# Layer 2's first step: five VectorE instructions and two ScalarE instructions change places

## The reference, cut to what matters

```python
x = attn_out.reshape(B * S, D)
h = x @ w_in;  g = h * np.cos(h);                          x = g @ w_out   # layer 1
h = x @ w_in2; g = h * np.clip(h + 3.0, 0.0, 6.0) / 6.0;   y = g @ w_out2  # layer 2
```

## Time and profile before

| | us |
|---|---|
| median of 3 runs | 1143.38 (1143.23 to 1143.67) |
| the profiled execution's own time | 1142.86 |
| its span, first to last instruction | 1140.9 |
| TensorE busy in the span | 1134.9 (99%) |
| ScalarE busy | 874.7 (77%) |
| VectorE busy | 808.4 (71%) |
| GpSimd busy | 786.5 (69%) |

### The profile page before, as it was taken

One profiled execution on the slowest core, in us unless ns is written; L12 is line 12 of the kernel. 1 busy time (PEld: TensorE's weight loads), 2 busy tenths in 40 slices (PEclk: granted clock), 3 DMA queues, 4 the chain that ended last, 5 costly groups with the idle time before them and its releaser, 6 DMA issues.

```text
span 1140.9 us, 16262 instructions
## 1 busy us (share of the span) xinstructions
PE 1134.9 (99%) x5350; PEld 960.9 (84%) x5350; DVE 808.4 (71%) x1120; ACT 874.7 (77%) x1457; POOL 786.5 (69%) x644
## 2 busy tenths in 40 slices
PE   9999999999999999999999999999999999999998
PEld 9888899888888888888888878888888888888898
DVE  6777856878888888888888887755555555555544
ACT  4777777778888888888889978767667677676665
POOL 0677677877868768768668999857557558557554
PEclk9999999999999999999999999999999999999999
DMA  9476465010020020020021210100100200200100
GB/s 348 120 226 188 144 208 195 15 48 9 1 74 1 1 74 1 1 74 1 18 76 56 91 59 1 38 37 1 61 14 1 75 1 1 70 1 1 38 1 32
DMA packets 44685, 68.47 MB, mean 60 GB/s; under 512 B 3497, under 2 KB 26761, under 8 KB 44602
## 3 DMA queue, kind: packets, MB, share of 16 engines
q1 hardware_dynamic: 44602, 67.43, 17.7%
HBM read 43.04 MB, written 24.48 MB: 59 GB/s over the span
## 4 chain that ended last, share of the span: by engine, by line
PE 97%; ACT 1%; DVE 1%; DMA 1%; issue 0%; SPq 0%; ACTq 0%; DVEq 0%
PE banks L762 41%; PE banks L740 36%; PE banks L698 3%; PE banks L718 3%; PE banks L669 2%; PE banks L612 2%; PE banks L617 2%; PE banks L613 2%; PE banks L575 2%; PE banks L636 1%; PE banks L633 1%; DMA xb<-in_x 1%; PE banks L639 0%; PE banks L651 0%; PE banks L652 0%; PE banks L654 0%
## 5 line engine op out<-in xcount | busy, mean ns | idle before, releaser
L1610 POOL TENSOR_TENSOR gb_lo<-gb,gbh 128x512 fp32r<-128x512 f32 (+1 forms) x352 | 465.4, 1333 | 264.1 <-ACT gbh L1120 261.5
L1120 ACT ACTIVATE gbh<-gb 128x512 fp32r<-128x512 f32 (+1 forms) x352 | 218.8, 621 | 74.1 <-DVE gb L1348 61.1
L762 PE MATMUL banks<-gbh,w1h 128*128 128x512 f32 (+1 forms) x704 | 272.5, 387 | 0.0
L762 PE MATMUL banks<-gb_lo,w1h 128*128 128x512 f32 (+1 forms) x704 | 272.5, 387 | 0.0
L762 PE MATMUL banks<-gbh,w_lo 128*128 128x512 f32 (+1 forms) x704 | 272.4, 387 | 0.0
L1348 DVE SCALAR_TENSOR_TENSOR gb<-gb,banks 128x512 f32<-128x512 f32 (+1 forms) x144 | 97.0, 673 | 134.9 <-ACT gb L1113 134.9
L762 PEld LDWEIGHTS banks<-gbh,w1h 128*128 128x128 f32 x704 | 132.1, 188 | 26.2 <-issue 0.3
L762 PEld LDWEIGHTS banks<-gb_lo,w1h 128*128 128x128 f32 x704 | 132.2, 188 | 25.9
L762 PEld LDWEIGHTS banks<-gbh,w_lo 128*128 128x128 f32 x704 | 132.1, 188 | 25.9
L1107 ACT ACTIVATE gb<-gb,half_pi 128x512 f32<-128x512 f32 x160 | 115.1, 720 | 33.8 <-DVE gb L1335 33.1
L740 PE MATMUL banks<-th,sh 128*128 128x512 f32 (+1 forms) x352 | 136.5, 388 | 0.0
(11 more groups left out here) (133 smaller groups left out, 2153.2 us busy)
## 6 DMA issues: line engine op xcount, KB each, us to landing
t<-x_spill SPq DMA_DIRECT2D x20, 512.0 KB, 4.7
w<-in_w_ff SPq DMA_DIRECT2D x32, 256.0 KB, 3.5
v<-y_spill SPq DMA_DIRECT2D x24, 260.0 KB
xb<-in_x SPq DMA_DIRECT2D x12, 512.0 KB, 9.8
dbs<-in_db SPq DMA_DIRECT2D x24, 256.0 KB, 2.7
y_spill<-y SPq DMA_DIRECT2D x24, 256.0 KB, 2.3
x_spill<-yt SPq DMA_DIRECT2D x10, 512.0 KB, 3.3
out_y<-yt SPq DMA_DIRECT2D x10, 512.0 KB, 3.1
```

What stands on the lines that cost most here:

```text
L762: mm = pe.matmul(bank[:, y_bank(tile) + c, 0:w], wt[:, at:at + P], a[:, 0:w], start=(p == 0 and e == 0 and n == 0), stop=(p == PAIRS - 1 a ...
L1120: act.activation(gbh[n % RING_H][:, 0:w], gb[n % RING_G][:, 0:w], ACT.Copy).then_inc(b_gh, 1)
L1610: pool.tensor_tensor(gbl[n % RING_G][:, 0:w], gb[n % RING_G][:, 0:w], gbh[n % RING_H][:, 0:w].bitcast(fp32), ALU.subtract).then_inc(b_gl, 1)
```

## The change

It touches ScalarE's and VectorE's lists in step 40 (CHANGE) and, through the deferral, ScalarE's step 41. No instruction is added or taken out. VectorE: c12 and c22 come ahead of gate 0, and the four output copies come between gate 1 and gate 2. ScalarE: round_gb(40,2) and take_ramp(40,3) come after keep_u5(41).

```diff
@@ -1191,6 +1191,9 @@
                 if s == CHANGE:
                     take_cos2(s - 1, 3)
                 keep_u5(s)
+                if s == CHANGE + 1:
+                    round_gb(CHANGE, 2)
+                    take_ramp(CHANGE, 3)
                 prepare2(s)
                 round_gb(s - 1, 3)
                 if s > CHANGE:
@@ -1200,8 +1203,9 @@
                 take_ramp(s, 1)
                 take_ramp(s, 2)
                 round_gb(s, 1)
-                round_gb(s, 2)
-                take_ramp(s, 3)
+                if s > CHANGE:
+                    round_gb(s, 2)
+                    take_ramp(s, 3)
             round_gb(STEPS2 - 1, 3)
 
 
@@ -1477,16 +1481,22 @@
                     down_low2(0)
                 if q == DUOS1 and 1 <= p < PAIRS - 1:
                     s_low2(p + 1)
-                take_gb(s, 0)
+                if s > CHANGE:
+                    take_gb(s, 0)
                 take_c12(s)
                 take_c22(s)
+                if s == CHANGE:
+                    take_gb(s, 0)
                 take_gb(s, 1)
-                take_gb(s, 2)
+                if s > CHANGE:
+                    take_gb(s, 2)
                 if p == 0:
                     take_y(q - 1, 0)
                     take_y(q - 1, 1)
                     take_y(q - 1, 2)
                     take_y(q - 1, 3)
+                if s == CHANGE:
+                    take_gb(s, 2)
                 take_gb(s, 3)
                 prepare2(s)
             for i in range(4):
```

## The result

The changed kernel took 1145.47 us in the median of 14 runs (1143.17 to 1146.65); the kernel before took 1143.41 us in 14 runs beside it (1141.83 to 1145.69). The ratio is 1.0015, with a 95% interval of 1.0008 to 1.0022: slower by 1.7 us (0.9 to 2.5). That is 0.15%, under the 0.2% that I had called the limit, and yet the interval lies clear of no change. The forecast was plus 1.0 us. The median stands 0.3 us over the top of the range (1145.2); the ratio applied to 1143.38, from which I had forecast, gives 1145.1.

What follows compares the result with a forecast made beforehand. TensorE, busy 1134.9 of 1140.9 us, was taken to bound the kernel. With 1.91 + 0.11 us lost and 0.73 + 0.12 + some 0.15 won, plus 1.01 on 1143.38 gave 1144.4 us; range 1142.8 to 1145.2.

Steps and rivals of the forecast that it cites:

- The two gaps: TensorE's waits at A22 of step 40 and down(0,0) of step 41 go: minus 0.73 and minus 0.12 us.
- Gate 2 behind gb_low(40,1): VectorE's gate 2 of step 40 starts 0.15 us behind GpSimd's gb_low(40,1), is held, and ends at 663.66.
- Rival 1: Gate 2 of step 40 starts first and ends at 662.66; S3 stops 0.8 us; time 1143.3 to 1143.8; chance 0.20.
- keep_u2 and the stop at S3: Step 41: ScalarE's keep_u2 ends at 667.47, so TensorE's S3 stops 1.91 us, plus 0.11 for the restart.
- A22 of step 41: Due at 670.36 with no further stop, against 669.35 before: plus 1.01 us at that point.
- Rival 3: s_low2(2) loses to gb_low(40,3), so A22 of step 41 stops 0.35 + 0.11 us; plus 1.5, 1144.9; chance 0.12.
- From step 42 the lists are those of before ... so the shift stays: From step 42, 0.7 us in hand at keep_u2 again, so the plus 1.01 us stays as it is.
- rival 4: Late gate 2 of step 41 makes keep_u2 of step 42 repeat the 2.02 us stop; plus 3.0, 1146.4; chance 0.04.
- Rival 2: New waits are covered; gain between 0.44 and 1.07 us, time 1142.3 to 1142.9; chance 0.12.
- The floor of 0.45 us: Least stop at S3 of step 41: ScalarE needs 4.26 us from S1's product, TensorE is there after 3.91; latencies included.
- The most that can be won is 1.07 us: TensorE's excess in steps 40 and 41, 0.79 + 0.28 us, taken as the limit of any gain.

Runs made afterwards that it cites:

- Experiment 4: Changed kernel with GpSimd's w2_low(2) moved behind gb_low(40,2); 491.63 us from step 40's first matmul to the end, 0.75 under the changed kernel.
- Experiment 3: Kernel before with only ScalarE's part of the change; 491.50 us from step 40's first matmul to the end, against 490.94 before.
- experiment 5: Changed kernel, step 41's keep_u2 ahead of the three weight roundings and gate 3's rounding; 492.61 us from step 40's first matmul to the end, against 492.38.
- Experiment 6: Changed kernel with one subtraction of step 41 moved from GpSimd to VectorE; 492.40 us from step 40's first matmul to the end, against 492.38.
- experiment 1: Kernel before with only c12 and c22 ahead of gate 0 in step 40; 490.98 us from step 40's first matmul to the end, against 490.94.
- experiment 2: Changed kernel with ScalarE's list as before; 494.10 us from step 40's first matmul to the end, 493.10 when run again, against 490.94 before.
- Experiment 7: Kernel before, nothing deferred: c12, c22 early in steps 40 and 41, tile 0's copies first, step 41's s_low2(2) later, keep_u2 sooner; 491.53 us from step 40, against 490.94.
- experiment 9: Experiment 7's kernel with two subtractions moved from GpSimd to ahead of gate 3 on VectorE; 490.57 us from step 40's first matmul to the end.

## Why the prediction held, and where it was short

- **The two gaps** (minus 0.73 and minus 0.12 us): both went, as the rows of after show.
- **Gate 2 behind gb_low(40,1)**: right. Forecast end 663.66, which is 665.42 on the scale of after; measured 665.45. The Trainium skill's page "SBUF — State Buffer" (section "SBUF: two separate sides") has it that the one that starts first keeps the shared ports for its whole instruction. The trace agrees: 0.56 us after GpSimd's end once more. Experiment 4 shows the cause: with GpSimd idle there the gate takes 0.68 us and S3's stop shrinks by just the 1.16 us. Rival 1, that gate 2 starts first, missed by less than the 0.15 us that I had: by 0.03 us, since VectorE came to the gate 0.12 us sooner than forecast. My working could not decide so small a distance, so that part was luck. Yet in all six profiles with this order (two of the change, two of VectorE's part alone, experiments 5 and 6) it was gate 2 that was held, for 1.80 to 1.84 us, with the recorded starts 0.00 to 0.05 us apart.
- **keep_u2 and the stop at S3**: forecast start of S3 667.53, so 669.29; measured 669.30. The stop was 1.91 us in the forecast, 1.93 measured. Experiments 3 and 5 show that the deferral needs the late gate to cost this much, and that keep_u2 was not the only late thing: c22 was next, 0.4 us from stopping A22 in the change.
- **A22 of step 41**: forecast plus 1.01 us, so 672.12; measured 672.15. Steps 40 and 41 together took 22.47 instead of 21.47 us, the forecast 1.0. Rival 3 (a second stop at A22) did not happen: s_low2(2) started at 668.55, 0.29 us ahead of gb_low(40,3) at 668.84.
- **"From step 42 the lists are those of before ... so the shift stays"**: this step of the prediction failed. It put the time behind step 41 at nothing, and that was 0.3 to 0.4 us. The small stop of 0.23 + 0.08 us in step 43 is new; one of 0.11 us in step 45 was 0.06 before. GpSimd's list came out of the stop late. ScalarE's rounding of gate 3, which stands behind the deferred pair, moved from 664.82 to 668.15, 1.57 us beyond the 1.76, and GpSimd's low part waits for it. So gb_low(41,0) starts at 672.13 and not at 669.04 + 1.76 + 1.04 = 671.84, where it would be if it were late by as much as A22 (672.15 against 669.35). That 0.29 us is not made up, as GpSimd is busy for 10.12 of step 42's 10.20 us.

  In step 43 VectorE's s_low2(4) (687.24) then starts ahead of gb_low(42,1) (687.49) and holds it to 687.49 + 1.75 = 689.24, when TensorE was due at 688.92 + 0.23 = 689.15. In the kernel before it was the other way round: gb_low(42,1) went first and took 1.30 us, and s_low2(4) took 1.75. Experiment 6 bears this out: with one operation less ahead of it on GpSimd the stop in step 43 is gone. Experiment 3 has the stop and the same order (s_low2(4) at 687.18 there, gb_low(42,1) at 687.38), and experiments 1 and 2, which defer nothing, don't: the stop came with the deferral.

  GpSimd's timeline of the kernel before, in step 43:

```profile
684.38 1.30 POOL L1610 TENSOR_TENSOR gb_lo<-gb,gbh 128x512 fp32r<-128x512 f32 x1
```

And VectorE's of the kernel before:

```profile
684.48 1.75 DVE L1366 TENSOR_TENSOR s_lo<-s,sh 128x512 fp32r<-128x512 f32 x1
```

  I had named GpSimd's full list as rival 4's ground, with a price of 3.0 us at keep_u2; it decided at another place, for 0.3.
- **Rival 2** (new waits covered) did not happen, and not in experiment 4 either: with the lock out of the way S3 still stops for 0.77 + 0.11 us. That is about the price that I had put on rival 1 (0.8 us; its own terms put the end of keep_u2 at 666.47 and not at 666.41). The floor of 0.45 us wants no wait for gate 2 at all, and 0.77 less ScalarE's idle 0.23 us is 0.54; no run has it by itself.
- **"The most that can be won is 1.07 us"** was true of TensorE's idle time and still too much. Experiment 7 removed 0.85 us of it, and GpSimd gave back more. The gaps of steps 40 and 41 had been its time to catch up; with two operations moved off GpSimd (experiment 9) steps 42 and 43 give back 0.51 us instead of 1.33.

The tail's plus 1.3 to 1.5 us and the runs' plus 1.7 us (0.9 to 2.5) agree within the interval. What the rest of the runs' difference is stays open, but TensorE's clock may have a part in it: six of the changed kernel's 14 runs have a mean granted clock of 0.998 or 0.999, and their median is 1146.2 us, against 1144.4 of the other eight. The profiled one of the six had 0.79 between 8 and 16 us from the start, where the kernel before had 1.00, long ahead of what the change touches. For the 14 runs of the kernel before beside it, the clock is not on record.

## What to carry to other kernels

Before a wait is taken out where three engines work by lists, play their lists on from that point with the rows' start-to-start times until every one of them has met its old slack again, the fullest engine above all: a gap of the critical engine may be the slack of another one. And when an operation with two SBUF inputs on VectorE moves, look which GpSimd operation is under way at its new place; here the gate came 0.03 us behind one and took 1.16 us more for it.

## What the hardware showed that I had not expected

TensorE's granted clock fell to 0.53, the lower of its levels (1.2 GHz) for nearly all of the stretch, for 3.5 us in one execution, from 1.0 us behind the end of a stop of 2.58 us, and the tail was 1.0 us longer than in the other execution of the same kernel, where it stayed at 1.00 behind a stop of 2.54 us at the same place. Stops of 1.89 and 1.93 us left it at 1.00. What decides is open. And which of VectorE and GpSimd is held turns on small lags: 0.29 us on GpSimd's side changed it in step 43, a step that the change does not touch.
